# A delta-rule layer with two feed-forward layers on one core: warming matmuls between the fills of the first stage, and other places in the order for Gram fills and weight cuts

## The reference

```python
for t in range(S):
    y[:, :, t] = einsum('bhd,bhde->bhe', q[:, :, t], state)
    v_old = einsum('bhde,bhd->bhe', state, k_n[:, :, t])
    state = state + beta_t * einsum('bhd,bhe->bhde', k_n[:, :, t], v[:, :, t] - v_old)
x = y as 3072 tokens x 384
h = maximum(x @ w_in, 0);  x = h * h @ w_out             # 384 -> 2048 -> 384
x = (sigmoid(x @ w_gate) * (x @ w_val)) @ w_out2         # 384 -> 1536 -> 384
```

## Time and profile before

| | |
|---|---|
| three runs | 1154.64 us median (1151.81 to 1157.68) |
| profiled execution | 1154.64 us; span from first to last instruction 1152.9 us |
| PE busy | 1041.9 us (90%) |
| DVE busy | 587.7 us (51%) |
| ACT busy | 439.0 us (38%) |
| mean granted PE clock | 0.933 |

### The profile page before, as it was taken

The page is one execution under the profiler, slowest core; times in us unless marked ns, Lnnn a source line. Parts: engine busy times, 40 slices in busy tenths (PEclk is TensorE's granted clock), DMA queues, the critical chain, the costliest instruction groups (busy, mean ns, idle before and its releaser), DMA issues.

```text
span 1152.9 us, 22982 instructions
## 1 busy us (share of the span) xinstructions
PE 1041.9 (90%) x9885; PEld 559.0 (48%) x9885; DVE 587.7 (51%) x1100; ACT 439.0 (38%) x752; POOL 12.6 (1%) x27
## 2 busy tenths in 40 slices
PE   2487589889988998899889999999999999999997
PEld 1285256446644664466446544444444444444443
DVE  7857944792489159716952445424233342422422
ACT  4544145425434443445244498222222222132221
POOL 0000000000000000000000000000000000000000
PEclk7559689988989998899889999999999999999999
DMA  9414002300230042004200050101001010010000
GB/s 299 74 43 71 0 2 46 67 28 2 71 42 29 2 94 45 1 16 70 110 2 2 1 193 27 55 1 55 0 0 55 0 55 0 0 55 0 27 0 27
DMA packets 54850, 48.10 MB, mean 42 GB/s; under 512 B 45424, under 2 KB 49392, under 8 KB 54384
## 3 DMA queue, kind: packets, MB, share of 16 engines
q1 hardware_dynamic: 54336, 46.67, 15.9%
q10 hardware_dynamic: 432, 0.23, 0.1%
HBM read 37.45 MB, written 9.44 MB: 41 GB/s over the span
## 4 chain that ended last, share of the span: by engine, by line
PE 74%; DVE 21%; issue 2%; ACT 1%; DMA 1%; SPq 0%; DVEq 0%; POOL 0%; POOLq 0%
PE psum L525 59%; DVE attn L875 4%; DVE attn L873 4%; DVE attn L893 3%; PE psum L401 3%; PE psum L463 2%; PE psum L476 2%; PE psum L436 2%; PE psum L451 2%; PE psum L413 2%; DVE work L915 2%; DVE work L934 1%; PE psum L425 1%; DVE attn L880 1%; DVE attn L834 1%
## 5 line engine op out<-in xcount | busy, mean ns | idle before, releaser
L525 PE MATMUL psum<-work,w 128*128 128x512 f16 x1728 | 411.0, 395 | 34.6 <-DVE work L915 30.5
L525 PE MATMUL psum<-work,attn 128*128 128x512 f16 x1944 | 419.9, 379 | 0.1
L525 PEld LDWEIGHTS psum<-work,attn 128*128 128x128 f16 x1944 | 190.1, 98 | 229.8 <-DVE work L934 0.6
L525 PEld LDWEIGHTS psum<-work,w 128*128 128x128 f16 x1728 | 167.3, 101 | 245.5 <-DVE work L915 39.0
L606 ACT ACTIVATE work<-work 128x512 f16<-128x512 f32 (+1 forms) x264 | 156.2, 624 | 147.2 <-DVE work L1096 139.9
L1096 DVE SCALAR_TENSOR_TENSOR work<-psum,work 128x512 f32<-128x512 f32 x72 | 49.8, 692 | 269.7 <-PE psum L525 258.8
L606 ACT ACTIVATE attn<-psum 32x512 f32<-32x512 f32 (+4 forms) x168 | 81.5, 500 | 107.5 <-PE psum L401 54.8
L606 ACT ACTIVATE work<-psum 128x512 f32<-128x512 f32 x96 | 57.0, 594 | 152.1 <-PE psum L525 151.8
L915 DVE SCALAR_TENSOR_TENSOR work<-work 128x512 f16<-128x512 f16 x96 | 66.2, 690 | 85.2 <-ACT work L606 83.8
L606 ACT ACTIVATE work<-psum,scal 128x512 f32<-128x512 f32 x72 | 49.4, 687 | 138.5 <-PE psum L525 137.8
L909 DVE TENSOR_TENSOR attn<-attn,psum 64x384 f32<-64x384 f32 x48 | 26.5, 552 | 86.4 <-PE psum L476 68.0
(11 more groups left out here) (77 smaller groups left out, 584.9 us busy)
## 6 DMA issues: line engine op xcount, KB each, us to landing
attn<-in_kt SPq DMA_DIRECT2D x24, 192.0 KB, 4.1
attn<-in_v SPq DMA_DIRECT2D x6, 768.0 KB, 4.8
attn<-in_kn SPq DMA_DIRECT2D x6, 768.0 KB, 7.4
x_spill<-work SPq DMA_DIRECT2D x6, 768.0 KB, 3.6
xt<-x_spill SPq DMA_DIRECT2D x6, 768.0 KB, 4.9
y_out<-work SPq DMA_DIRECT2D x6, 768.0 KB, 3.6
attn<-in_qt SPq DMA_DIRECT2D x20, 192.0 KB, 4.7
work<-in_w_out SPq DMA_DIRECT2D x1, 3072.0 KB, 21.6
```

What stands on the lines that cost most here:

```text
L525: m = mm(dst, x, z, start=first and i == 0, stop=last and i == len(a) - 1)
```

## The change

It moves the four `kk` fills of stage 0 from step 27 to steps 24, 24, 25, 25, so ahead of the last two `xt` (26); moves the second and third piece of w_in's cuts from steps 14 and 20 to 21 and 24; moves the four pieces of w_out's cuts from steps 20, 24, 24, 24 to 25, 26, 28, 28 (28 being the step of the reduction L919); queues two matmuls of `keep_clock` ahead of each of the 30 fills of stage 0; and makes the `keep_clock` behind stage 0 24 matmuls instead of 12.

```diff
-KK_AT, KK_FIRST_AT = (12, 14, 16, 18), (27, 27, 27, 27)
+KK_AT, KK_FIRST_AT = (12, 14, 16, 18), (24, 24, 25, 25)
...
-FIRST_IN_AT, FIRST_OUT_AT = (9, 14, 20), (20, 24, 24, 24)
+FIRST_IN_AT, FIRST_OUT_AT = (9, 21, 24), (25, 26, XMAX_AT, XMAX_AT)
 SMALL_AT = (OFF_AT, DR_AT[0], XT_AT[0], DR_AT[1])
-WARM_START, WARM_MID, WARM_END = 11, 14, 12
+WARM_START, WARM_MID, WARM_PIECE, WARM_END = 11, 14, 2, 24
...
                         if kind == "mid" and x == 0:
                             pe.wait_ge(lane_step, L_ROWS - 10)
                             keep_clock(WARM_MID)
+                        keep_clock(WARM_PIECE)
                     if kind in ("kk", "qk"):
```

## The result

Five timed runs of the changed kernel have a median of 1165.63 us (1162.77 to 1166.9), five of the kernel before 1156.11 us. The ratio is 1.0084 with a 95% interval of 1.0065 to 1.0103: slower by 0.84%, some 9.5 us. The forecast was 1156.3 us, in a range of 1149.5 to 1164.

The account below looks back on a forecast made before the run. PE bounds the whole kernel, but DVE's exit from stage 0 at 105.38 us shifts everything behind it. Full-clock terms summed to +0.1 us, a short clock fall added 1.5: 1156.3 us on 1154.64, range 1149.5 to 1164.

Parts of the forecast that it names:

- The clock: Stage 0 near 52 us: falls to half again, returns after about 3.5 us of pairs and fills, +1.5 us.
- Rival (b): Stage 0 clock returns late: near 73 us with the solves, +8.9, 1163.5, chance 0.10; near 62, +4.5, 1159.1, chance 0.13.
- Rival (a): Clock never falls at 52 us, as the first pair shortens the idle time: +0.1, 1154.8 us, chance 0.22.
- The pair's price: Two warming matmuls ahead of 29 stage 0 fills lie in PE's path: 29 x 0.46 = 13.3 us at full clock.
- The sum: Stage 0 at full clock: fills 29.2, pairs 13.3, waits 0.7, then DVE's work; handover at 105.5, +0.1 us against 105.38.
- The bound "up to 0.1 a fill, +3": Changing between full-array and small matmuls in stage 0 may add up to 0.1 us a fill, +3 us.
- The waits: PE's 3.09 us wait at L463 becomes 0.4, all waits 0.7 instead of 3.7; DVE idle 1 to 2 us ahead of L919.
- Kk and the cuts: Stage 0: kk goes ahead of the last turn, costing 3.9 us; two w_out cuts put 3.5 between L919 and scale.
- Behind stage 0: From DVE's L834 to PE's L413 again 45.7 us, and everything behind it unchanged.
- Rival (d): Pairs cost nothing in stage 0 because PE would have waited there: -8 to -10 us, about 1146.5, chance 0.09.

Follow-up runs that it names:

- e1: The changed kernel run once more, nothing altered: 1164.99 us, 1.0086 of before.
- e10: Changed kernel with kk at 27, cuts at 9, 15, 20 and 20, 20, 20, 24, 28 matmuls ahead of first mid, no pairs, 12 at end: 1145.4 us.
- e11: The kernel before with 28 instead of 14 full-width matmuls ahead of the first mid, nothing else: 1152.62 us, 0.9971.
- e6: The changed kernel with all cuts of w_in and w_out back in their old places: 1163.4 us, 1.0065 of before.
- e7: The changed kernel with 28 instead of 14 full-width matmuls ahead of the first mid and no pairs: 1152.8 us, 0.9966 of before.
- e4: The changed kernel with 26 instead of 14 full-width matmuls ahead of the first mid, pairs kept: 1159.71 us, 1.0039 of before.
- e12: The changed kernel with four instead of two full-width matmuls ahead of each fill: 1170.51 us, 1.0119 of before.
- e2: The changed kernel with kk and all cuts back in old places, keeping pairs and the 24 at the end: 1159.74 us, 1.0033 of before.
- e3: The changed kernel with the moves alone, no pairs and 12 matmuls at the end: 1156.4 us, 0.9999 of before.
- e8: The changed kernel with 28 full-width matmuls ahead of the first mid, no pairs, kk back at 27: 1151.76 us, 0.9965 of before.
- e5: The changed kernel with only kk of group 1 back at step 27: 1161.15 us, 1.0052 of before.
- e9: Changed kernel with kk at 27, cuts at 9, 15, 20 and 20, 20, 20, 24, bridged first mid, one matmul a fill, 12 at end: 1145.74 us.

## Why the prediction was wrong

- **The clock, the step that failed.** It was put as "I take it that the clock falls there again and is back after about 3.5 us of pairs and fills: +1.5". It does fall there, and comes back after 20.5 us (e1), and that costs 8.6. The price per us at half clock was right: a pair with its fill takes 1.61 us at full and 2.85 at half in the two profiles, so 1 - 1.61/2.85 = 0.43 for 0.44 forecast. Only how long it stays at half was wrong, and no row of before spoke for 3.5 us. The row that did bear on it was read and set aside: small matmuls at half clock, without a pause, had not raised the clock in 10 us, and two thirds of PE's time were to remain that work. Later profiles show returns as short as the forecast one and much longer ones, of pieces with and without pairs: 3.4 us at half in e10 and in e11, 17 and 7 in e6, 24 in e7. What decides the length stays open. The idle time wasn't 0.5 us shorter than the 2.25 of before either, but longer, 2.53 and 3.27 us, since the clock rose earlier in these executions.
- **Rival (b)**, late return, had 0.10 for "they end near 73 on a half-speed path ... +8.9: 1163.5", against 73.2 us and 1165.5 measured. The moment and the time are its own; its reason, that the solves raise the clock, is not borne out: in e6 full speed is back at 68.3, ahead of any solve. So the agreement is in part luck.
- **Rival (a), 0.22**: the clock isn't lost. It is the first profile, one execution of fifteen. Its reason was a shorter idle time ahead of L413. e4, with none, keeps the clock in its profile, but of idle times between 2 and 3.3 us the length doesn't sort the cases: the clock held at 1.96 (e12) and 2.53, and fell at 2.25 (before), 2.41 (e6), 2.81 (e2) and 3.27 (e1). What decides between them stays open.
- **The two parts of the loss.** DVE's handover is 2.4 us later than before at full clock (107.78 against 105.38) and another 8.6 where the clock falls, 11.0 in all; the times of those executions, 1165.5 and 1154.64, are 10.9 apart. The five runs give 9.5, their kernel before being at 1156.11. So even without the fall the change would not have been a gain: e4 is 3.9 us above the kernel before.
- **The pair's price.** The sum took 0.46 us at full clock; between small fills it is 0.53, and 0.44 ahead of a turn. For 29 pairs that is 15.2 us for 13.3, with 0.1 of waiting in it. The sum gave 105.5 for DVE's handover and the full-clock profile has 107.78, so with this term the rest of it holds to 0.4 us, in part because two errors cancel: the 30 fills take 29.9 us for 29.2 (a Gram fill 1.08 for 0.97, a turn 0.43 for 0.55), and of 0.7 us of waits only that 0.1 is left. The bound "up to 0.1 a fill, +3" held it, but the sum should have stood there.
- **The waits.** The wait at L463 is gone, as forecast (0.4, none seen). L920's idle time was forecast as 1 to 2 us and is 2.48.
- **Kk and the cuts.** Their places were right in the sum, but the prediction didn't price them by themselves, and it booked the shorter wait (3.0 us) as a gain that only the move gives. Combined with pairs the moves cost 5.2 us (e2 against e1), alone nothing (e3). By the profiles the cuts' places cost 3.7 us behind the last state update in both, and give something back ahead of it only where there is a wait to remove (1.6 us in e3); at e2's half clock the pairs had filled it. Kk's place costs 2.3 us with pairs and nothing without (e7 against e8): a kk without its pair is a third shorter, so DVE's own cuts cover it. At full clock in the middle of the stage a part of the wait would be left, as the 1.89 us ahead of the first L463 in e6 show, so how much the move gives there isn't measured.
- **Behind stage 0**: 45.7 or 45.8 us from L835 to L413 and 1001.5 to 1001.8 behind, in the profiles of before, of the changed kernel and of e1, as forecast. In the other profiles the time from DVE's handover to the end wanders from 1046.2 (e5) to 1049.5 (e11), against 1047.3 to 1047.5 in these three, so differences of 1 or 2 us between medians can come from there.
- **Rival (d)**, that pairs hide in waits: nothing shows it. The full-clock profile has all 29 pairs in PE's path with no waits but 0.1 us, and e7 without them is 6.9 us faster than e4 with them. Pairs are seen to fill a wait in e2 alone, at half clock.

## What to carry to other kernels

Filler matmuls between fills are in the path wherever the engine doesn't wait, so reckon them against what the clock gives back there: here two a fill cost 15 us, where 20 us at full instead of half clock are worth 9. Filler in idle time costs little: 28 matmuls ahead of L413 left 0.25 to 0.71 us of idle time in e8, e9 and e11 and overran it in e4, e7 and e10, by 0.7 us at most (e7), since they take longer when the clock rises later. With it the clock was still full 6 us behind L413's start in all six profiles that have it, and it had fallen by then in all but two of the eight without. How long it stays at half after that varies from 3 to 24 us. And before moving an engine's background work behind its last result, look for an earlier wait of the same engine that is long enough: that was worth about 6 us here (e8 to e10), more than all that was done for the clock (3.4 us, e11).

## What the runs showed of the hardware

- The same work was seen at either level of the clock. Pairs between small fills went with a full clock for 45 us (first profile, 51.5 to 96.6), and the same instructions left it at half for 20.5 us in e1 with PE busy for all of the time. One profile (e6) has it back after 17 us of them, ahead of any solve, so the solves are not what it needs. Nor are pairs: in e10 it came back after 3.4 us of small matmuls alone (65.3 to 68.7). What it needs stays open.
- The Trainium skill (TensorE: Matmul & The Clock Gate, Part 1) says that the moment of the transition varies from run to run for the same kernel. The runs agree: near 45.9, 47.0, 47.5, 47.8 and 47.9 us in e1, e2, the first profile, e6 and e12, with the first full-width matmul at 43.2 to 43.4 in each. An early rise makes the idle time at 50 us longer, but it doesn't explain the fall behind it: the clock fell in e1 (rise at 45.9) and in e6 (47.8), and held in the first profile (47.5).
- A profile is one execution. The first profile of the changed kernel was one in fifteen, and its span alone (1155.1 against 1152.9) would have confirmed the forecast. The mean granted clock of the timed runs was what gave it away. That mean is a hint and no more: e5's profile has 0.945 with 20.5 us at half in stage 0, e4's has 0.946 with none.
- Two full-width matmuls take 0.46 us in a row of their own, 0.53 between small fills at full clock and 0.97 at half; four take 0.97 between small fills at full clock (e12).
